# Attention scores of two heads side by side in the TensorE array, a VectorE step between two search rounds, a fourth w1 buffer

## The reference

```python
# 1 attention that keeps the 32 largest scores of each row
scores = (1 / sqrt(64)) * q @ k.transpose(0, 1, 3, 2)
kth = np.partition(scores, -32, axis=-1)[..., -32:-31]
scores = np.where(scores >= kth, scores, -1e9)
scores = scores - scores.max(-1, keepdims=True)
attn = exp(scores); attn /= attn.sum(-1, keepdims=True) + 1e-9
x = (attn @ v)                      # then (4, 576, 512)
# 2 gated block
gate_pre = sum(conv_w[k] * shifted(x, k) for k in range(5))   # causal, 5 taps
x = (sigmoid(gate_pre) * (x @ w_val)) @ w_out
# 3 Fourier mixing and feed-forward
u = x + real(fft(fft(x, axis=1), axis=2))
un = (u - mean(u)) / sqrt(var(u) + 1e-6)
out = u + relu(un @ w_ch1) @ w_ch2                            # 512 -> 2048 -> 512
```

## Time and profile before

| | us |
|---|---|
| median of 3 runs (lowest, highest) | 1087.59 (1083.38, 1087.86) |
| the profiled execution, own time | 1088.74 |
| its span | 1086.7 |
| PE busy (matmul) | 987.4 (91%) |
| DVE busy | 829.1 (76%) |
| ACT busy | 633.4 (58%) |
| POOL busy | 377.7 (35%) |

### The profile page before, as it was taken

One profiled execution on the slowest core, in us unless ns is written; L12 is line 12 of the kernel. 1 busy time (PEld: TensorE's weight loads), 2 busy tenths in 40 slices (PEclk: granted clock), 3 DMA queues, 4 the chain that ended last, 5 costly groups with the idle time before them and its releaser, 6 DMA issues.

```text
span 1086.7 us, 19607 instructions
## 1 busy us (share of the span) xinstructions
PE 987.4 (91%) x6624; PEld 810.0 (75%) x6624; DVE 829.1 (76%) x1809; ACT 633.4 (58%) x1397; POOL 377.7 (35%) x520
## 2 busy tenths in 40 slices
PE   4877766899989999899999999999889999999997
PEld 3556555786778888775988888776778887668896
DVE  7999999998998998969988887889989943120000
ACT  5777887655666766546676755656666661122211
POOL 2575554223333332224342323234432122243221
PEclk9987988899999999989999999999999999999999
DMA  8556657020568777200877665220676774239874
GB/s 246 169 167 208 222 196 242 24 73 22 169 216 266 274 270 270 92 22 13 311 259 247 211 214 196 77 62 23 206 263 236 263 249 148 78 121 356 297 247 150
DMA packets 81186, 200.35 MB, mean 184 GB/s; under 512 B 8384, under 2 KB 26560, under 8 KB 81088
## 3 DMA queue, kind: packets, MB, share of 16 engines
q1 hardware_dynamic: 80928, 198.81, 54.3%
q10 hardware_dynamic: 160, 0.30, 0.1%
HBM read 177.58 MB, written 21.50 MB: 183 GB/s over the span
## 4 chain that ended last, share of the span: by engine, by line
PE 66%; DVE 19%; issue 6%; ACT 4%; DMA 2%; POOL 1%; SPq 1%; DVEq 0%; ACTq 0%; POOLq 0%
PE p_m L659 17%; PE p_m L673 16%; PE p_m L546 14%; DVE rest L879 9%; DVE top L885 7%; PE p_t L535 6%; PE p_s L505 5%; PE p_t L519 5%; DMA w_st<-w_split 2%; DVE top L870 1%; PE p_t L539 1%; ACT pT L763 1%; PE p_m L598 1%; ACT prob L749 1%; PE p_m L644 1%
## 5 line engine op out<-in xcount | busy, mean ns | idle before, releaser
L885 DVE MAX8 top<-rest 128x8 f32<-128x576 f32 x432 | 304.3, 745 | 0.0
L1116 POOL TENSOR_TENSOR hid_lo<-hid,hid_hi 128x256 fp32r<-128x256 f32 (+1 forms) x128 | 105.0, 820 | 319.3 <-ACT hid_hi L822 319.3
L879 DVE MATCH_REPLACE8 rest<-top,rest 128x576 f32<-128x576 f32 x288 | 211.4, 741 | 0.0
L659 PE MATMUL p_m<-un_hi,w_st 128*128 128x256 f32 (+1 forms) x1024 | 166.4, 306 | 19.0 <-ACT hid_hi L822 7.4
L673 PE MATMUL p_m<-w_st,hid_hi 128*128 128x512 f32 x576 | 182.1, 397 | 0.7 <-POOL hid_lo L1116 0.7
L659 PEld LDWEIGHTS p_m<-un_hi,w_st 128*128 128x128 f32 x1024 | 143.4, 191 | 31.2 <-issue 20.9
L737 ACT ACTIVATE s_sb<-p_s 128x576 f32<-128x576 f32 x144 | 93.2, 647 | 105.0 <-PE p_s L505 104.7
L519 PE MATMUL p_t<-id_sb,prob 128*128 128x128 f32 x720 | 109.8, 286 | 29.2 <-ACT prob L755 29.2
L821 ACT ACTIVATE hid<-p_m 128x256 f32<-128x256 f32 (+1 forms) x128 | 51.3, 401 | 142.5 <-PE p_m L659 142.5
L505 PE MATMUL p_s<-k_hi,q_st 128*128 128x288 f32 x320 | 109.9, 359 | 18.3 <-ACT s_sb L737 9.1
L535 PE MATMUL p_t<-pT,v_sb 128*64 128x128 f32 (+1 forms) x1600 | 108.8, 287 | 19.4 <-ACT pT L763 19.4
(11 more groups left out here) (99 smaller groups left out, 1543.4 us busy)
## 6 DMA issues: line engine op xcount, KB each, us to landing
w_st<-w_split SPq DMA_DIRECT2D x256, 512.0 KB, 4.5
w_split<-w_st SPq DMA_DIRECT2D x32, 512.0 KB, 3.2
k_raw<-kT SPq DMA_DIRECT2D x62, 144.0 KB, 3.0
q_raw<-qT SPq DMA_DIRECT2D x60, 144.0 KB, 2.9
u<-w_ch SPq DMA_DIRECT2D x32, 256.0 KB, 4.0
v_sb<-v SPq DMA_DIRECT2D x16, 256.0 KB, 3.2
wslot<-w_val SPq DMA_DIRECT2D x4, 1024.0 KB, 7.6
wslot<-w_out SPq DMA_DIRECT2D x4, 1024.0 KB, 5.3
```

Of the source, the lines that this page charges most:

```text
L659: mm = pe.matmul(mbank(HIDDEN_BANK[g], n), w1_st[i % NB1][:, w, k, :], x[:, k, at:at + n], start=part + k == 0, stop=part + k == KC + 1)
L879: dve.match_replace(rest[tt % 2][:, :], top[tt % NK][:, 8 * n - 8:8 * n], src[:, :], LOWEST).then_inc(s_chain, 1)
L885: found = dve.max(top[tt % NK][:, 8 * n:8 * n + 8], rest[tt % 2][:, :])
```

## The change

The change has five parts.

1. Scores. `q_hi`, `q_lo`, `k_hi` and `k_lo` now hold both heads of a pair, head 0 in partitions 0 to 63 and head 1 in 64 to 127. Tile 2j of a unit is now both heads against the first 288 keys, tile 2j + 1 both heads against the other 288, in three terms (high times high, low times high, high times low): six matmuls of 64 rows by 128 columns, by turns in the upper and lower rows, each head into its own PSUM bank. Tile 8 keeps 128 rows (the left queries are padded with zeros in the other head's rows) and has six matmuls in place of eight.
2. Score buffers. `s_sb` (6 tiles) becomes `s_all` (4 units of 2 tiles). A row of scores is complete only when both tiles of its unit are copied, so `select` waits for the copies of the whole unit.
3. Splits and loads. A pair is loaded by four DMAs on SP, two of them 64 x 64, all at slot 7, and split by one ACT and one POOL instruction for q and one each for k (slots 0 to 3 of the pair before), where there were five on ACT and five on POOL.
4. VectorE runs a slot's first step between rounds 2 and 3 where the slot has them.
5. `NB1` goes from 3 to 4.

```diff
-NS = 6
-FILLS = 18
+FILLS = 15
+NU = 4
+WHOLE = (S // P) * P
+QW = WHOLE + P
-LOAD = {8: 0, 4: 1}
-HIGH_Q, HIGH_K, LOW_Q, LOW_K = {0: 0, 5: 1}, {1: 0, 6: 1}, {2: 0, 6: 1}, {3: 0, 7: 1}
+LOAD_AT = 7
+HIGH_Q, LOW_Q, HIGH_K, LOW_K = 0, 1, 2, 3
+HIGH_Q0, LOW_Q0, HIGH_K0, LOW_K0 = 2, 3, 4, 5
-NB1, NB2 = 3, 3
+NB1, NB2 = 4, 3
...
+        def unit_tiles(n):
+            p, j = divmod(n, 5)
+            return TILES * p + min(2 * j + 2, TILES)
+        def scores_of(t):
+            return s_all[:, unit_of(t) % NU, tile_of(t)[1] % 2, :]
+        def copies_upto(t):
+            return unit_tiles(unit_of(t))
...
+                def load_keys(p):
+                    if p:
+                        sp.wait_ge(s_lo, 2 * p)
+                    b, p = divmod(p, PAIRS)
+                    sp.dma_start(k_raw[:, :], kT[b, 2 * p:2 * p + 2].rearrange("h d n -> (h d) n")).then_inc(s_k_in, 16)
...
                 def scores(t):
                     p, i = tile_of(t)
-                    heads = [0, 1] if i == TILES - 1 else [i % 2]
-                    for h in heads:
-                        pe.wait_ge(s_lo[h], (2 + h) * (p + 1))
+                    if i == 0:
+                        pe.wait_ge(s_lo, 2 * (p + 1))
                     if t:
                         pe.wait_ge(s_copy, t)
-                    cols = slice(P * (i // 2), P * (i // 2) + P)
-                    for o in range(2):
-                        parts = [(h, k[h][p % 2]) for h in heads for k in (k_hi, k_lo)]
-                        for n, (h, k) in enumerate(parts):
-                            mm = pe.matmul(p_s[:, o, 0:HALF_S], q_st[h][p % 2][:, cols],
-                                           k[:, o * HALF_S:o * HALF_S + HALF_S], start=n == 0,
-                                           stop=n == len(parts) - 1)
+                    terms = [(q_hi[p % 2], k_hi[p % 2]), (q_lo[p % 2], k_hi[p % 2]), (q_hi[p % 2], k_lo[p % 2])]
+                    if i == TILES - 1:
+                        for o in range(2):
+                            for n, (q, k) in enumerate(terms):
+                                mm = pe.matmul(p_s[:, o, 0:HALF_S], q[:, WHOLE:QW], k[:, o * HALF_S:o * HALF_S + HALF_S],
+                                               start=n == 0, stop=n == 2)
+                    else:
+                        o, c0 = i % 2, P * (i // 2)
+                        for n, (q, k) in enumerate(terms):
+                            for h in range(2):
+                                at = slice(D * h, D * h + D)
+                                mm = pe.matmul(p_s[:, h, 0:HALF_S], q[at, c0:c0 + P],
+                                               k[at, o * HALF_S:o * HALF_S + HALF_S], start=n == 0, stop=n == 2)
                     mm.then_inc(s_qk, 1)
...
                         for tt in tiles:
-                            dve.wait_ge(s_copy, tt + 1)
+                            dve.wait_ge(s_copy, copies_upto(tt))
...
-                    if due(s, SELECT + 1) and (s - SELECT - 1) % 2:
+                    second = due(s, SELECT + 1) and (s - SELECT - 1) % 2
+                    if second:
                         select(s - SELECT - 1, 1)
...
+                        for x in plan[s][0:1]:
+                            step(*x)
+                        select(s - SELECT - 1, 2)
                     for b, c, taps in conv_due(s):
                         conv(b, c, taps)
-                    for x in plan[s]:
+                    for x in plan[s][1:] if second else plan[s]:
                         step(*x)
```

More of the change, by code:

```diff
@@ L241, in build @@
         s_feat_ev = sem("s_feat_ev")
-        s_qk_in = [sem(f"s_qk_in{h}") for h in range(2)]
+        s_q_in = sem("s_q_in")
+        s_k_in = sem("s_k_in")
         s_v_in = [sem(f"s_v_in{i}") for i in range(2)]
-        s_hi = sem("s_hi")
-        s_lo = [sem(f"s_lo{h}") for h in range(2)]
+        s_qhi = sem("s_qhi")
+        s_khi = sem("s_khi")
+        s_lo = sem("s_lo")
         s_qk = sem("s_qk")
@@ L309, in due @@
             return 0 <= s - lag < ALL_TILES
-        def raw(p, h):
-            if p == 0 and h == 1:
-                return x_new[NX - 2][:, TAPS - 1:XW], x_new[NX - 1][:, TAPS - 1:XW]
-            return q_raw[:, :], k_raw[:, :]
+        def unit_tiles(n):
[5 more added lines that the diff above has]
+            return unit_tiles(unit_of(t))
         def split_at(s, first, others):
             p, i = divmod(s, TILES)
-            h = (others if p else first).get(i)
-            return (p + 1, h) if h is not None and p + 1 < ALL_PAIRS else None
+            return p + 1 if i == (others if p else first) and p + 1 < ALL_PAIRS else None
         def unit_due(s):
@@ L448, in step @@
                                     sp.dma_start(out[bb, c0:c0 + m, :], u_row(bb, r)).then_inc(m_put, 16)
-                for half in range(2):
-                    sp.dma_start(k_raw[D * half:D * half + D, :], kT[0, 0]).then_inc(s_qk_in[0], 16)
-                load_qk(0, 1)
+                load_keys(0)
+                sp.wait_ge(s_zero, 1)
+                load_left_queries(0, sp)
                 sp.wait_ge(s_zero, FILLS)
@@ L467, in _ @@
                     p, i = divmod(s, TILES)
-                    ahead = p + 2 - LOAD.get(i, 0)
-                    if i in LOAD and ahead < ALL_PAIRS:
-                        load_qk(ahead, LOAD[i])
+                    if i == LOAD_AT and p + 2 < ALL_PAIRS:
+                        load_queries(p + 2)
+                        load_keys(p + 2)
                     i = part_due(s, 1)
@@ new lines, in high_keys, with copy_scores @@
+                def high_keys(p):
+                    act.wait_ge(s_k_in, 16 * (p + 1))
+                    if p >= 2:
+                        act.wait_ge(s_qk, TILES * (p - 1))
+                    act.activation(k_hi[p % 2][:, :], k_raw[:, :], ACT.Copy).then_inc(s_khi, 1)
+                def copy_scores(t):
+                    p, i = tile_of(t)
+                    n = unit_of(t)
+                    act.wait_ge(s_qk, t + 1)
+                    if n >= NU and i % 2 == 0:
+                        act.wait_ge(s_drop, unit_tiles(n - NU))
+                    if i == TILES - 1:
+                        to = s_all[:, n % NU, 0, :].rearrange("p (o n) -> p o n", o=2)
+                    else:
+                        to = s_all[:, n % NU, :, HALF_S * (i % 2):HALF_S * (i % 2) + HALF_S]
+                    act.activation(to, p_s[:, :, 0:HALF_S], ACT.Copy, scale=SCALE).then_inc(s_copy, 1)
@@ L748, in exponent @@
                         act.wait_ge(s_tr, t - 2)
[L749 removed]
+                    act.activation(prob[t % 3][:, 0:S], scores_of(t), ACT.Prelu,
                                    bias=kth, scale=-1.0, alpha=1.0 / BIG).then_inc(s_drop, 1)
```

144 lines of the change are left out of this document (48 added, 96 removed).

## The result

The changed kernel takes 1090.62 us in the median of 20 runs (1088.91 to 1092.03), the kernel before 1088.37 us in 20 runs of the same chip (1083.01 to 1091.51). The ratio is 1.0024, with a 95% interval of 1.0013 to 1.0036: 2.6 us slower, which is less than the 0.5% named above. The forecast was 1092.4 us. Within one kernel the time goes with TensorE's granted clock (its mean over a run): the kernel before, run 23 times beside one set of experiments, took 1082.2 us at 0.974 and 1094.0 us at 0.962, and all 20 runs of the changed kernel have 0.959 or 0.962.

The account below looks back on a forecast made before the run. DVE's search bounds 11 to 187 us, PE the rest. Terms 11.3 - 5.5 - 1.5 - 1 + 0 + 0.5 + 1 = +4.8 us on 1088.74 give 1093.5, less 1.15 to the median: 1092.4 us, range 1086 to 1100.

Parts of the forecast that it names:

- The scores: Score matmuls on PE, slots 43 to 143: row halves run side by side, but array shape changes cost more; +11.3 us.
- The loads of w1: PE's 5.5 us of waits for w1, 187 to 870 us, go with the changed load order; -5.5 us, between -5.5 and 0.
- The moved step: DVE step ahead of round 3: the 1.55 us idle before `hidden` at 516.18 goes; -1.5 us, between -4 and +2.
- Lighter ACT and POOL: ACT has three instructions fewer a pair, against PE's 6.6 us wait for the exponential; -1 us, between -5 and 0.
- The start: Kernel start: `k_hi` starts sooner, but q's POOL split and two copies keep round 1 at about 13.3 us; 0.
- The first stage: 11 to 187 us, DVE-bound search: whole-unit wait is tight in one place, at 137.26 us; +0.5 us, up to +4.
- The wait for the whole unit in the second stage: Late score copies delay 13 of 24 searches, but DVE's 69 us idle hides nearly all; +1 us, between 0 and +13.
- The second stage: 187 to 870 us: PE busy 651 of 683 us, so time added to PE counts whole unless idle places absorb it.
- A: Rival: the heads' row halves do not run side by side, or their weight loads queue; 1119 to 1127 us, chance 0.16.
- B: Rival: changes of the array's shape cost nothing in practice; scores give -13.8 us, time 1067 us; chance 0.17.
- C: Rival: the whole-unit wait puts DVE on the path from 187 to 870 us; 1104 us, chance 0.11.
- D: Rival: the waits for w1 are the landing itself, not SP's order, and stay; 1098 us, chance 0.09.

Follow-up runs that it names:

- run 23: Not a run's label: the unchanged kernel before, executed 23 times beside one set of experiments; 1082.2 us at clock 0.974, 1094.0 us at 0.962.

## Why the prediction was right

The time was 1.8 us from the forecast, inside the forecast's own range of 1086 to 1100, and the change is slower by less than 0.5%. The prediction gave more chance to a loss above 0.5% (0.53) than to this (0.26). The mechanism that was to decide it is what happened: the halves run side by side, and the changes of shape cost more than they save. But that the number came so close is luck: one term was missing, another was put at nearly nothing, and they have opposite signs.

- **The scores, +11.3 us: right.** The rows give +0.21 us for a tile in a stream, as predicted, and +0.015 us behind `attend` for +0.02; with tile 8 at −0.26 us the sum is 66 × 0.21 + 23 × 0.015 − 3.1 = +11.1 us, and the table has +10.0 us (638.3 for 628.3). The pair at 0.13 us, taken over from column halves, holds for row halves. The prediction's 0.33 us for a change round measured 0.35 us. The Trainium skill (TensorEngine Tiling (Array Packing), Key Properties) says that a change of tiling mode drains TensorE and that different tiles can load weights and multiply in parallel; the trace agrees, with 0.35 us for the one and 0.13 us a pair for the other.
- **The loads of w1, −5.5 us: the waits were sized right, the clock was not in the sum.** They go in the changed kernel, and a fourth buffer in the kernel before takes 5.0 us of idle time away. The gain there is some 10 us (9.8 by the ratio, 10.3 in the profile), the other half being the clock. "Between −5.5 and 0" was a wrong bound: I took the sum of the waits that the view names for the most that could be had.
- **The moved step, −1.5 us: right,** 1.4 us in the profile, at the place that was named.
- **Lighter ACT and POOL, −1 us:** not tested alone. The wait that it was to shorten stayed (6.8 us for 6.6).
- **The start, 0: off by a little.** Scores start at 7.58 us in place of 8.39, the first MAX8 at 11.22 us, and the first MATCH_REPLACE8 stands at 12.62 us, where 13.31 was read before.
- **The first stage, +0.5 us: this step failed.** Slot 42 came 6.6 us late. The prediction looked there for one thing, the wait for the whole unit at 137.26 us, and that wait alone delays the search by 0.9 us. What it left out: the change round is paid in this stage too. PE, whose granted clock is lowest there, and ACT pass work to each other, and a tile's copy comes late by the sum. A window of the changed kernel, and where DVE then stands still:

```profile
90.00:130.00 40.00, 29.54 (x209) 23.20 (x209) 40.00 (x84) 29.84 (x62) 17.28 (x22) 0.67 0.51 172
```

```profile
170.45 0.76 DVE L893 MAX8 top<-s_all 128x8 f32<-128x576 f32 x1 [2.90 <-ACT s_all L764]
```

The clock is 0.67 there (0.79 before), and DVE waits 2.90 us for one copy, behind 1.20 us for one at 138.51 us. With that the search of tile 35 ends 3.6 us late, at 189.2 us. The other 3 us come behind it on PE; the kernel before with four w1 buffers has slot 42 at +4.2 us with its search on time (+0.4 us), so they can come without the new scores. The opening sentence had the condition ("only if DVE comes to wait for it"), but the sum charged the scores from slot 43 on alone. With three full matmuls the loss goes (+0.5 us at slot 42, the search on time); with the halves one after the other it grows to 21.7 us. How much of it the whole-unit wait adds once the copies are late is open: both were changed together, and no run here parts them.
- **The wait for the whole unit in the second stage, +1 us: right.** DVE waits 14.7 us there, and PE waits no more for the exponential than before. In the kernel before, alone, the ratio stands for +1.4 us.

The second stage measured −4.4 us, and the table gives its parts: +10.0 us of work, −7.5 us of idle time and −6.8 us for 13.7 us less at 1.2 GHz. The prediction had +11.3 us of work and −7.0 us of waits (−5.5, −1.5, −1 and +1), which is +4.3 us, and no term for the clock. Against it the second stage's error was −8.7 us, nearly all of it the clock, and the first stage's was +6.1 us, and they cancelled. What made PE fall to 1.2 GHz less often there no run isolates.

Of the rivals, A (one after the other) is excluded: that kernel takes 1137 us. B's condition does not hold. Its time, 1067 us, is nearly what the kernel without changes of shape takes, 1068 us, and its −13.8 us for the scores are −15.1 us in the table (613.2 for 628.3). C did not come: DVE waits, PE doesn't. D fell with the waits for w_st.

## What to carry to other kernels

Packing two small contractions into halves of the array pays only if it saves more than about 0.35 us for each time the array goes to halves and back, which here is nearly three matmuls of 288 columns: put many packed matmuls together, or put them beside others that are packed already, and look first at what else that order had been covering. A wait in a view is not the bound of what its removal gives: look at the granted clock of the same stretch too, before a gain or a loss is put down to an edit. A cost on PE has to be asked about in each stage, also in the one where another engine seems to be the bound. A change made of five parts should be taken apart: here the parts that gained, alone in the kernel before, give 1077.3 us, and the part with the most new code took all of it back.

## What the runs showed of the hardware

- Two matmuls of 64 rows in the two row halves start 3 to 10 ns apart and cost one (0.13 us for 288 columns), weight loads included; on the same half they cost two (0.13 us more a pair, 1137 us in all).
- At 1.2 GHz PE's work takes twice as long: twenty matmuls of `attend` last 2.40 us where they last 1.31. Six kernels with the same matmuls and 6.8 to 20.5 us at 1.2 GHz have 628.1 to 629.0 us of busy time once half of that is taken off.
- The two halves do not keep the program's order between them: issued as three for head 0 and then three for head 1, they still start in twos (362.14, 362.37, 362.50 us). The Trainium skill (TensorE: Matmul & The Clock Gate, The mechanism) says that matmuls start in the program's order; the trace does not agree here, and the measurement decides.
- A change to row halves and back costs 0.35 us in a stream of full matmuls: 0.10 us ahead of the first pair, 0.10 us between the first and the second, 0.09 us ahead of the transposes and 0.05 us behind the first of them. Beside column halves it is 0.15 us.
